# Gate rows of a chunk in five parts: chunk 1's around the first hidden products with its low row on GpSimd, chunks 2 and 3 later in block zero

## What is computed

```python
for t in range(S):                       # per batch and head
    m_new = maximum(f[t] + m, i[t])
    f_stab, i_stab = exp(f[t] + m - m_new), exp(i[t] - m_new)
    C = f_stab * C + i_stab * outer(v[t], k[t]);  n = f_stab * n + i_stab * k[t]
    y[t] = sigmoid(o[t]) * (C @ q[t]) / maximum(abs(n @ q[t]), 1)
x = (sigmoid(x @ w_gate) * (x @ w_val)) @ w_out            # layer 0, x = y as (1536, 320)
xn = x / sqrt(mean(x * x) + 1e-6) * rms_g
out = (silu(xn @ w_gate2) * (xn @ w_val2)) @ w_out2        # layer 1
```

## Time and profile before

| | us |
|---|---|
| median of 3 runs | 497.21 (497.19 to 497.32) |
| the profiled execution, its own time | 494.57 |
| its span (first to last instruction) | 492.8 |
| PE busy | 481.4 |
| DVE busy | 237.4 |
| ACT busy | 196.4 |
| POOL busy | 110.6 |

### The profile page before, as it was taken

One profiled execution on the slowest core, in us unless ns is written; L12 is line 12 of the kernel. 1 busy time (PEld: TensorE's weight loads), 2 busy tenths in 40 slices (PEclk: granted clock), 3 DMA queues, 4 the chain that ended last, 5 costly groups with the idle time before them and its releaser, 6 DMA issues.

```text
span 492.8 us, 8606 instructions
## 1 busy us (share of the span) xinstructions
PE 481.4 (98%) x3443; PEld 467.1 (95%) x3443; DVE 237.4 (48%) x516; ACT 196.4 (40%) x406; POOL 110.6 (22%) x146
## 2 busy tenths in 40 slices
PE   8699899999999999999999999999999999999997
PEld 4699799999999999999999999999999999999997
DVE  7926973643558246426434626540554055405540
ACT  4467818341653456153515744321232123212320
POOL 7857941111111101110004997000000000000000
PEclk9879999999999999999999999999999999999999
DMA  7662530122021102100240530001000100010001
GB/s 258 229 212 81 147 105 13 44 70 59 27 59 44 44 29 61 53 1 2 97 145 9 177 122 1 1 1 40 1 0 2 41 0 1 0 41 2 0 1 40
DMA packets 11470, 27.83 MB, mean 56 GB/s; under 512 B 1526, under 2 KB 5830, under 8 KB 11430
## 3 DMA queue, kind: packets, MB, share of 16 engines
q1 hardware_dynamic: 11110, 27.20, 17.4%
q10 hardware_dynamic: 320, 0.08, 0.1%
HBM read 25.23 MB, written 1.97 MB: 55 GB/s over the span
## 4 chain that ended last, share of the span: by engine, by line
PE 92%; DVE 3%; ACT 3%; issue 1%; DVEq 0%; ACTq 0%
PE bank L926 20%; PE bank L927 20%; PE bank L929 13%; PE bank L947 9%; PE bank L949 9%; PE bank L948 9%; PE bank L871 4%; PE bank L844 2%; PE bank L957 2%; PE bank L800 1%; PE bank L863 1%; PE bank L881 1%; PE bank L819 1%; PE bank L821 1%; ACT L552 1%
## 5 line engine op out<-in xcount | busy, mean ns | idle before, releaser
L926 PE MATMUL bank<-x_hi,wgv_hi 128*128 128x256 f32 (+1 forms) x720 | 219.2, 310 | 4.1 <-DVE x_lo L711 4.1
L927 PE MATMUL bank<-x_lo,wgv_hi 128*128 128x256 f32 (+1 forms) x720 | 215.6, 305 | 0.0
L929 PE MATMUL bank<-x_hi,wgv_lo 128*128 128x256 f32 (+1 forms) x480 | 146.4, 305 | 0.0
L926 PEld LDWEIGHTS bank<-x_hi,wgv_hi 128*128 128x128 f32 x720 | 138.0, 192 | 5.9 <-DVE x_lo L711 4.3
L927 PEld LDWEIGHTS bank<-x_lo,wgv_hi 128*128 128x128 f32 x720 | 138.1, 192 | 0.4
L552 ACT ACTIVATE sg<-bank 128x256 f32<-128x256 f32 (+1 forms) x120 | 51.0, 426 | 162.2 <-PE bank L927 161.9
L756 DVE TENSOR_TENSOR hf<-sg,bank 128x256 f32<-128x256 f32 (+1 forms) x120 | 56.7, 473 | 73.2 <-ACT sg L552 70.3
L929 PEld LDWEIGHTS bank<-x_hi,wgv_lo 128*128 128x128 f32 x480 | 91.9, 191 | 0.0
L947 PE MATMUL bank<-wo_hi,h_hi 128*128 128x320 f32 x288 | 89.6, 311 | 0.0
L949 PE MATMUL bank<-wo_hi,h_lo 128*128 128x320 f32 x288 | 89.0, 309 | 0.0
L948 PE MATMUL bank<-wo_lo,h_hi 128*128 128x320 f32 x288 | 89.0, 309 | 0.0
(11 more groups left out here) (107 smaller groups left out, 438.4 us busy)
## 6 DMA issues: line engine op xcount, KB each, us to landing
step<-in_w_gv SPq DMA_DIRECT2D x7, 576.0 KB, 3.7
step<-in_vok SPq DMA_DIRECT2D x12, 324.0 KB, 3.3
step<-in_qk_t SPq DMA_DIRECT2D x24, 160.0 KB
raw_x<-in_w_gv SPq DMA_DIRECT2D x5, 576.0 KB, 4.9
raw_p<-in_w_gv SPq DMA_DIRECT2D x4, 576.0 KB, 5.3
y<-y_tok SPq DMA_DIRECT2D x12, 160.0 KB, 1.8
step<-in_vok SPq DMA_DIRECT2D x10, 180.0 KB, 4.1
step<-in_q_t SPq DMA_DIRECT2D x10, 180.0 KB, 2.5
```

Source lines behind the costliest of these rows:

```text
L926: pe.matmul(ps, wgv_hi[:, wc, s, cs], x_hi[:, xs, s, :], start=(s == 0), stop=False)
L927: mm = pe.matmul(ps, wgv_hi[:, wc, s, cs], x_lo[:, xs, s, :], start=False, stop=(s == 2))
L929: pe.matmul(ps, wgv_lo[:, wc, s, cs], x_hi[:, xs, s, :], start=False, stop=False)
```

## The change

`rows` now has five subs: 2 is L635, L636 and the rounded `l_row` (raising a new semaphore `high_done`), 3 is the remainder into `d_lhs` (raising a new `lhs_done`) and, except for chunk 1, the remainder of `l_row` (`rows_done`), 4 is `l_end`. For chunk 1 the remainder of `l_row` is made by POOL, between `split(0, 0)` and `split(0, 1)`. Chunk 1's sub 2 stands ahead of the S pieces, sub 3 behind the T pieces and sub 4 behind the K pieces. ACT issues F(1) ahead of T(0) and T(1). D(n) on PE waits for `lhs_done` as well. For chunks 2 and 3, sub 1 moves from slot 8 to slot 10 of block 0, sub 2 from slot 10 to slot 12, and subs 3 and 4 to slot 13; F(2) moves from slot 12 to slot 14, behind T(3). For chunks 4 and 5 the end of the rows moves from slot 7 to slot 9 of block 2.

```diff
-         [("A", 2, 1)], [("S", 3), ("T", 2)], [("A", 2, 2)], [("K", 3), ("N", 3)], [("Y", 3), ("F", 2)], [],
-         [("T", 3)], [("R", 2)]]
+         [], [("S", 3), ("T", 2)], [("A", 2, 1)], [("K", 3), ("N", 3)], [("Y", 3), ("A", 2, 2)], [("A", 2, 3), ("A", 2, 4)],
+         [("T", 3), ("F", 2)], [("R", 2)]]
...
             slots[7] += [("A", 3, 2)]
+            slots[9] += [("A", 3, 3), ("A", 3, 4)]
...
-            for c in range(4):
+            split(0, 0)
+
+            pool.wait_ge(high_done, 2)
+            pool.tensor_tensor(l_row[Q:Q + R, P:2 * P], l_r[:, P:2 * P], l_row[0:R, P:2 * P].bitcast(F32),
+                               ALU.subtract).then_inc(rows_done, 1)
+            pool.wait_ge(rows_done, 2)
+            for c in range(1, 4):
                 split(0, c)
...
             high(0, 2)
+            piece(("F", 1))
             piece(("T", 0))
             piece(("T", 1))
-            piece(("F", 1))
...
-                else:
+                elif sub == 2:
                     link(dve.tensor_tensor(i_r[:, cs], i_r[:, cs], l_r[:, cs], ALU.subtract))
                     dve.tensor_copy(d_lhs[2 * Q:2 * Q + R, cs], i_r[:, cs])
-                    link(dve.tensor_copy(l_row[0:R, cs], l_r[:, cs]))
+                    dve.tensor_copy(l_row[0:R, cs], l_r[:, cs]).then_inc(high_done, 1)
+                    dve.wait_ge(high_done, part + 1)
+                elif sub == 3:
                     dve.tensor_tensor(d_lhs[3 * Q:3 * Q + R, cs], i_r[:, cs], d_lhs[2 * Q:2 * Q + R, cs].bitcast(F32),
-                                      ALU.subtract)
-                    dve.tensor_tensor(l_row[Q:Q + R, cs], l_r[:, cs], l_row[0:R, cs].bitcast(F32),
-                                      ALU.subtract).then_inc(rows_done, 1)
...
+                                      ALU.subtract).then_inc(lhs_done, 1)
+                    if part != 1:
+                        dve.tensor_tensor(l_row[Q:Q + R, cs], l_r[:, cs], l_row[0:R, cs].bitcast(F32),
+                                          ALU.subtract).then_inc(rows_done, 1)
+                else:
...
             rows(1, 0)
             rows(1, 1)
+            rows(1, 2)
             for n in range(B):
                 piece(("S", n))
             for n in range(B):
                 piece(("N", n))
                 piece(("Y", n))
-            rows(1, 2)
             for n in range(B):
                 piece(("T", n))
+            rows(1, 3)
             for n in range(B):
                 piece(("K", n))
+            rows(1, 4)
...
                     else:
+                        pe.wait_ge(lhs_done, part_of(j) + 1)
                         pe.wait_ge(flat_in, 32 * j)
```

More of the change, by code:

```diff
@@ L221, in mlstm_moe_kernel @@
         selc_done = sem("selc_done")
+        high_done = sem("high_done")
         rows_done = sem("rows_done")
+        lhs_done = sem("lhs_done")
         flat_in = sem("flat_in")
@@ L633, in rows @@
                     link(dve.tensor_tensor(i_r[:, cs], i_r[:, cs], m_r[:, cs], ALU.subtract))
-                else:
+                elif sub == 2:
                     link(dve.tensor_tensor(i_r[:, cs], i_r[:, cs], l_r[:, cs], ALU.subtract))
                     dve.tensor_copy(d_lhs[2 * Q:2 * Q + R, cs], i_r[:, cs])
-                    link(dve.tensor_copy(l_row[0:R, cs], l_r[:, cs]))
+                    dve.tensor_copy(l_row[0:R, cs], l_r[:, cs]).then_inc(high_done, 1)
+                    dve.wait_ge(high_done, part + 1)
+                elif sub == 3:
                     dve.tensor_tensor(d_lhs[3 * Q:3 * Q + R, cs], i_r[:, cs], d_lhs[2 * Q:2 * Q + R, cs].bitcast(F32),
-                                      ALU.subtract)
-                    dve.tensor_tensor(l_row[Q:Q + R, cs], l_r[:, cs], l_row[0:R, cs].bitcast(F32),
-                                      ALU.subtract).then_inc(rows_done, 1)
[L642 to L647, removed]
+                                      ALU.subtract).then_inc(lhs_done, 1)
[3 more added lines that the diff above has]
+                else:
+                    dve.tensor_tensor(l_end[:, j0:j1, :, :],
+                                      l_r[:, lo + P - 1:hi:P].unsqueeze(2).unsqueeze(2).to_broadcast([R, j1 - j0, B, H]),
+                                      sel[0:R, :, :].unsqueeze(1).to_broadcast([R, j1 - j0, B, H]),
+                                      ALU.mult).then_inc(lend_done, 1)
             def weigh(n):
@@ L724, in _ @@
             link(dve.memset(d_lhs[0:Q + R, 0:P].bitcast(F32), 1.0))
-            for sub in range(3):
+            for sub in range(4):
                 rows(0, sub)
```

## The result

The changed kernel takes 491.49 us as the median of four runs (489.98 to 493.79), the kernel before 497.23; the ratio is 0.9888, 95% interval 0.9849 to 0.9927. So it is faster by 5.1 to 5.7 us, inside the range of the forecast, 2.3 us above its point. Each run also reports its mean granted clock of PE. The four runs spread over 3.8 us and go by it: 489.98 to 491.62 at 0.986 to 0.989, 493.79 at 0.983.

What follows compares the result with a forecast made beforehand. PE was taken as the bound, through its waits and its clock. Gains of 2.92 + 2.60 + 2.48 = 8.00 us took 497.21 to 489.2 us, range 488.2 to 492.0.

Steps and rivals of the forecast that it cites:

- the start: The change's first half, ahead of block 0: 2.92 us of wait plus 2.60 of clock, together 5.52 us.
- the tables: The change's second half, rows moved to later slots: removes PE's wait before K of step 3, 2.48 us.
- Part 1: First hidden product of block 0, waiting for `x_lo`: starts at 21.84 instead of 24.76, gaining 2.92 us.
- the first cover: Three row instructions put ahead of the S pieces: delay costs nothing up to 0.5 us, 0.3 at its upper end.
- E: Rival: chunk 1's split or step 1's y ends late, first product at 23.3 or later, clock down; 493.3 us, chance 0.03.
- Part 2: PE's clock in slots 0 and 1 of block 0: stays up, 3.82 instead of 6.42 us, gaining 2.60.
- rival B: Clock stays or falls low in slots 0 and 1: 491.8 us if whole, 490.5 if half; chance 0.18.
- The offset of 2.64 us: Runs without the profiler stand 2.64 us above the profiled execution; the distance was kept in the forecast time.
- Part 3: Slots 0 to 5: K of step 2 moves by 5.52 us and its wait stays 0.85; no further gain.
- Part 4: PE's wait before K of step 3 ends, gaining 2.48 us; the last `h_lo` is covered by 0.2 to 1.0.
- C: Rival: DVE late around slots 10 to 12 or ACT in slots 1 to 5; 490.0 to 491.7 us, chance 0.10.
- F: Rival, slower: ACT stands at F(1) waiting for POOL's low row, `x_hi` queued behind; about 498.2 us or more, chance 0.03.

Runs made afterwards that it cites:

- e2: The changed kernel's order ahead of block 0, with the slot tables of the kernel before: 497.51 us, ratio 1.0026.
- e1: The changed slot tables (blocks zero and two), with everything ahead of block 0 as in the kernel before: 491.62 us, ratio 0.9910.
- e9: The changed kernel with products of zeros on PE: 8 ahead of N, 2 between the two steps' N, 5 behind each T: 488.47 us.
- e7: The changed kernel with POOL's low row ahead of its two `vk` products, so POOL waits for chunk 1's roundings: 489.07 us, ratio 0.9834.
- e11: The changed kernel itself run once more beside the kernel before, with a second trace: 491.74 us, ratio 0.9905.
- e3: The changed kernel with eight products of zeros on PE between the S and N products: 490.48 us.
- e4: The changed kernel with chunk 1's two roundings on ACT, the low row one weight chunk later and F(1) behind `x_hi`: 491.04 us.
- e6: e4 with products of zeros on PE: 3 ahead of N, 2 between the two steps' N, 5 behind each T: 487.06 us.
- e10: The kernel before with products of zeros: 2 between the N, 2 and 16 behind the two T, ten ahead of K of step 3: 492.03 us.
- e5: The kernel before with ten needless products on PE in its wait ahead of K of step 3: 494.38 us, ratio 0.9960.
- e8: e7 with products of zeros on PE: 1 ahead of N, 2 between the two steps' N, 5 behind each T: 487.09 us.

## Why the prediction was right or wrong

**The time** was inside the range, at its upper part, and the sign was right. But the two halves of the sum were both mis-sized, in opposite directions: the start was given 5.52 us and brings nothing in the median (e2 against before, e1 against the changed kernel); the tables were given 2.48 and bring 5.2 (e1). The point missed by 2.3 us only because these nearly cancel.

**Part 1, the first product at 21.84: wrong.** The step that failed is the first cover, "the S pieces start 0 to 0.8 us late, most likely within 0.2", costed at nothing. They started 1.78 us late (1.2 in e2, 0.6 in e9). I had the row that says so, a CAST of 0.91 beside POOL, and set it aside because POOL has "only the `vk` multiplies there". Two of these and a weight split are just what three instructions of DVE ran beside and outlasted; with POOL held back they were short (e7). I also priced only the three moved instructions and not the scan ahead of them, which stands in the same stretch and lost 0.5 us. And the idle time of DVE ahead of the first y, which was to meet a delay, is the time in which it waits for N, and N waits for the S pieces: PE had nothing between the scores and N, so the delay became 2.00 us of idle PE.

The other three covers held: the low row took 0.45 (0.4 taken), F(1) on ACT went out at 16.57, D(2) didn't wait. Chunk 3's rounding, which was to start at 21.3, started at 25.71 behind the late `x_hi`, and no wait came of it. That E's chance was 0.03 was too low; what happened is E's mechanism, "step 1's y through later S pieces", with a larger price.

**Part 2, the clock: the number came, the mechanism failed.** The step was "With the shorter gap I take the clock to stay up". The gap ahead of block 0 shrank to 1.2 or 1.3 us in six traces (changed, e11, e2, e3, e4, e7), and in five of them PE was at 1.2 GHz through it and in slot 0. Only in the first trace of the changed kernel did slots 0 and 1 run at 2.4 GHz, in 3.95 us, because there the grant had fallen early, at 14.4, and had risen at 24.6, ahead of the gap; N took 3.15 us more than before instead. So the 2.60 that came true in the slots was luck, and over all the change won 1.5 us of clock, not 2.60. The row that I called a fall without a gap, 0.50 at 17 us, was the rule of this stretch, and it is rival B's. "The gap of 2.45 us that left it at 1.00" was one trace's luck, too: in e2 the same wait was followed by 10 us at 1.2 GHz. The rule that the prediction cited from the Trainium skill, "TensorE: Matmul & The Clock Gate", Part 1, that activity has to release the throttled state, fits the traces: each rise in the table came while PE worked or, once, 0.4 us behind its last product (e1), and with products of zeros in the waits and among the thin products there was no fall (e6, e9, e10).

**The offset of 2.64 us** between the profiled execution and the others was taken as a constant of measuring. It was the difference between the two groups of before, and so a cost that the second half of the change could remove; by e1 (5.2 us for a wait of 2.5) it did.

**Part 3 held**: the wait before K of step 2 stayed at 0.86, and at 0.84 to 0.86 in all other traces but e10's (0.63), whatever happened ahead of it; only the shift was 0.69 instead of 5.52.

**Part 4 held, and was undersized.** The wait went, no other came: sub 1 ended at 64.37 behind slot 10, the last `h_lo` at 67.05, and PE waited for nothing between 60 and 68 us. What it lacked is a term for the clock behind the wait, 2.3 us in the median (e5).

C and F did not occur. The lower end of the range was a small slip: with the 0.85 of part 3 gone as well the sum gives 488.4, not 488.2.

## What to carry to other kernels

Before small VectorE instructions are moved into a gap, look at what GpSimd does in those microseconds: three instructions of 0.2 to 0.4 us became 0.9 each, and each started behind a GpSimd instruction's start and ended just after that instruction did. Price a wait of TensorE with the clock behind it, and look for the clock in stretches of thin products even where there is no wait; and where times fall into groups, look at the grant of each run before the distance from the profiled execution is taken as fixed. If a wait can't be removed, some needless products in it can be worth more than the wait itself: here 4.8 us in the kernel before (e10), and 487.06 us for the best version (e6; e8 has 487.09), 1.9% less than before.

## What the hardware showed beyond that

The clock of TensorE can fall with no idle time at all: in e1 it fell 2.3 us into 32 products of 41 columns that followed each other without a gap, and they slowed from 0.12 us each (3.74 us for 32 at 1.00, in e3) to 0.22 (7.02 us for 32 at 0.50, in the changed kernel). Where it falls differs from run to run: the changed kernel's two traces have it at 14.4 and 16.1 us, with the same waits ahead of it. Once down, it stayed down for 3.4 us (the kernel before, its first fall) to 13.7 us (e4, e11), and for 10.2 us behind the wait in e2 though PE was busy all the time. What makes it fall at one place rather than another, and what brings it up again, these runs don't settle. In the kernel before, the mean grant of a run tells its time to about 1 us: 0.990 goes with 494.5 to 495.2 us, 0.979 to 0.986 with 496.5 to 497.7. In the changed kernel it is less sharp: runs at 0.989 lie between 489.98 and 491.77.
